# One PSUM copy of 576 columns for the ninth tile's turned rows and both heads' tails, and a chunk-by-chunk layout of pt

## The reference

```python
# attention: batch 4, 8 heads, 576 positions, head dimension 64
scores = scale * q @ k.T                       # scale = 1/8
thresh = max(scores, axis=-1) - tau
scores = where(scores >= thresh, scores, -1e9)
attn = exp(scores - max(scores)); attn /= sum(attn) + 1e-9
x = attn @ v                                   # -> 2304 tokens x 512
# first layer pair: h = x @ w_in (512 x 2048); g = s * relu(h)**2 + b; x = g @ w_out
# second layer pair: h = x @ w_in; g = max(h, 0) + alpha * min(h, 0); out = g @ w_out
```

## Time and profile before

| | us |
|---|---|
| median of three runs | 1088.46 (1088.38 to 1089.14) |
| the profiled execution's own time | 1089.1 |
| its span, first to last instruction | 1087.3 |
| TensorE busy | 1075.3 |
| VectorE busy | 526.4 |
| ScalarE busy | 505.9 |
| GpSimd busy | 257.3 |
| mean granted TensorE clock | 0.996 |

### The profile page before, as it was taken

The page is one execution under the profiler, slowest core; times in us unless marked ns, Lnnn a source line. Parts: engine busy times, 40 slices in busy tenths (PEclk is TensorE's granted clock), DMA queues, the critical chain, the costliest instruction groups (busy, mean ns, idle before and its releaser), DMA issues.

```text
span 1087.3 us, 18967 instructions
## 1 busy us (share of the span) xinstructions
PE 1075.3 (99%) x5826; PEld 892.6 (82%) x5826; DVE 526.4 (48%) x1017; ACT 505.9 (47%) x946; POOL 257.3 (24%) x438
## 2 busy tenths in 40 slices
PE   8999999999999999999999999999999999999998
PEld 7877877777788888888888889888888888888897
DVE  7988989888643332242242246522422332332232
ACT  4877878787754332232232235544433333333343
POOL 3666656666574200000000014322000000000000
PEclk8999999999999999999999999999999999999999
DMA  8666666565121100000000003211100100010010
GB/s 187 159 148 160 153 143 157 139 152 135 40 58 49 49 1 1 1 0 0 0 0 0 0 20 88 87 49 30 40 0 0 39 0 0 0 39 0 0 39 20
DMA packets 86554, 59.28 MB, mean 55 GB/s; under 512 B 49376, under 2 KB 69872, under 8 KB 86512
## 3 DMA queue, kind: packets, MB, share of 16 engines
q1 hardware_dynamic: 83248, 57.58, 20.6%
q10 hardware_dynamic: 3264, 1.18, 0.5%
HBM read 30.94 MB, written 4.72 MB: 33 GB/s over the span
## 4 chain that ended last, share of the span: by engine, by line
PE 91%; ACT 3%; DVE 2%; issue 2%; SPq 1%; DMA 0%; ACTq 0%; DVEq 0%
PE psum L947 23%; PE psum L948 23%; PE psum L949 23%; PE psum L1084 6%; PE psum L1050 5%; PE psum L976 3%; PE psum L978 3%; DVE act_r L883 2%; PE psum L1079 1%; ACT pt L645 1%; PE psum L960 1%; PE psum L1058 1%; ACT ex L623 1%; ACT win_hi L600 1%; SPq L434 1%
## 5 line engine op out<-in xcount | busy, mean ns | idle before, releaser
L947 PE MATMUL psum<-x_hi,win_hi 128*128 128x512 f32 (+1 forms) x640 | 235.7, 368 | 0.0
L948 PE MATMUL psum<-x_lo,win_hi 128*128 128x512 f32 (+1 forms) x640 | 235.5, 368 | 0.0
L949 PE MATMUL psum<-x_hi,win_lo 128*128 128x512 f32 (+1 forms) x640 | 235.5, 368 | 0.0
L947 PEld LDWEIGHTS psum<-x_hi,win_hi 128*128 128x128 f32 x640 | 120.7, 189 | 20.8 <-DVE x_lo L876 0.2
L948 PEld LDWEIGHTS psum<-x_lo,win_hi 128*128 128x128 f32 x640 | 120.6, 188 | 20.4
L949 PEld LDWEIGHTS psum<-x_hi,win_lo 128*128 128x128 f32 x640 | 120.7, 189 | 19.9
L894 DVE SCALAR_TENSOR_TENSOR act_r<-act_n,nalpha,act_r 128x512 f32<-128x512 f32 (+1 forms) x80 | 56.1, 702 | 155.6 <-ACT act_r L724 155.4
L883 DVE SCALAR_TENSOR_TENSOR act_r<-act_r,s_c 128x512 f32<-128x512 f32 (+1 forms) x80 | 73.1, 914 | 111.0 <-ACT act_r L713 111.0
L716 ACT ACTIVATE g_hi<-act_r,b_c 128x512 fp32r<-128x512 f32 (+1 forms) x80 | 54.5, 681 | 151.7 <-PE psum L949 121.6
L557 POOL TENSOR_SCALAR ex<-ex,none_in,rinv 128x576 f32<-128x576 f32 x142 | 117.1, 827 | 30.0 <-DVE rinv L814 29.2
L623 ACT ACTIVATE ex<-psum,negm 128x576 f32<-128x576 f32 x144 | 107.1, 747 | 29.2 <-DVE negm L795 28.1
(11 more groups left out here) (94 smaller groups left out, 1611.2 us busy)
## 6 DMA issues: line engine op xcount, KB each, us to landing
k_twice<-k_hi SPq DMA_DIRECT2D x64, 144.0 KB, 2.4
stage<-in_moe_w_out_dram SPq DMA_DIRECT2D x32, 256.0 KB, 2.6
out_dram<-stage SPq DMA_DIRECT2D x18, 256.0 KB, 2.2
q_both<-q_hi SPq DMA_DIRECT2D x32, 128.0 KB, 2.3
q_both<-q_lo SPq DMA_DIRECT2D x32, 128.0 KB, 2.3
win_raw<-in_moe_w_in_dram SPq DMA_DIRECT2D x16, 256.0 KB, 2.9
stage<-in_moe_w_in_dram SPq DMA_DIRECT2D x16, 256.0 KB, 2.7
raw_q<-in_q_dram SPq DMA_DIRECT2D x30, 128.0 KB, 2.4
```

The costliest lines, as they stand in the source:

```text
L947: nc.tensor.matmul(dst, lhs[0], rhs[0], start=first, stop=False)
L948: nc.tensor.matmul(dst, lhs[0], rhs[1], start=False, stop=False)
L949: return nc.tensor.matmul(dst, lhs[1], rhs[0], start=False, stop=final)
```

## The change

`turn_last` makes four transposes for the chunks as before, and two ordinary float32 matmuls against columns of the identity instead of the last two transposes. The first takes the tile's last 128 key columns as stationary operand and identity columns 64 to 127 as moving operand: it gives 128 x 64, and its partitions 64 to 127 are head 1's tail. The second takes the last 64 key columns and identity columns 0 to 63, gives 64 x 64, and overwrites partitions 0 to 63 with head 0's tail. The tails then stand as 64 columns right behind the 512 of the chunks, in the same partitions as in the destination. `copy_last` is one copy of 128 x 576.

For that, `pt` gets nine blocks of 576 columns, block `2 * c + h` for chunk `c` and head `h`, and block 8 for the tails; `pt_tails` is gone. `copy_turned` and `times_v` address the new layout. The 64 extra columns of `ex`, their memset and its count in `PADDED` are gone. Waits and semaphores are otherwise as before.

```diff
-        ex = sb("ex", [P, TPP * S + LAST], where=att)
+        ex = sb("ex", [P, TPP * S], where=att)
-        pt = sb("pt", [P, 2, QT - 1, S], where=att)
-        pt_tails = sb("pt_tails", [P, S], where=att)
+        PT_TAILS = 2 * (QT - 1)
+        pt = sb("pt", [P, PT_TAILS + 1, S], where=att)
...
-        PADDED = 7
+        PADDED = 6
...
                 if t.tails:
-                    dst = pt_tails[:, t.q0:t.q0 + 2 * P].rearrange("p (j q) -> p j q", q=P)
+                    dst = pt[:, PT_TAILS, t.q0:t.q0 + 2 * P].rearrange("p (j q) -> p j q", q=P)
                     nc.scalar.copy(dst, t.buf[:, 0:2, :]).then_inc(turned_out, 1)
                 else:
-                    nc.scalar.copy(pt[:, t.head, :, t.q0:t.q0 + P], t.buf).then_inc(turned_out, 1)
+                    dst = pt[:, 0:PT_TAILS, :].rearrange("p (c h) q -> p h c q", h=2)[:, t.head, :, t.q0:t.q0 + P]
+                    nc.scalar.copy(dst, t.buf).then_inc(turned_out, 1)
...
-                nc.scalar.copy(pt[:, :, :, S - LAST:S],
-                               t.wide[:, 0, :].rearrange("p (c h q) -> p h c q", h=2, q=LAST))
-                nc.scalar.copy(pt_tails[0:LAST, S - LAST:S], t.wide[0:LAST, 1, P:P + LAST])
-                nc.scalar.copy(pt_tails[LAST:P, S - LAST:S], t.wide[LAST:P, 1, LAST:P]).then_inc(last_out, 1)
+                src = t.wide.rearrange("p a c -> p (a c)")[:, 0:(PT_TAILS + 1) * LAST].rearrange("p (b q) -> p b q", q=LAST)
+                nc.scalar.copy(pt[:, :, S - LAST:S], src).then_inc(last_out, 1)
...
-            nc.vector.memset(ex[:, TPP * S:TPP * S + LAST], 0.0).then_inc(padded, 1)
...
-                for c in range(QT + 1):
-                    k0 = FULL * S + (c * P if c < QT - 1 else S - P if c == QT - 1 else S - LAST)
-                    dst = t.wide.rearrange("p a c -> p (a c)")[:, c * P:(c + 1) * P]
-                    mm = nc.tensor.transpose(dst, ex[:, k0:k0 + P], ident[:])
-                mm.then_inc(last_turned, 1)
+                end = FULL * S + S
+                for c in range(QT - 1):
+                    k0 = FULL * S + c * P
+                    nc.tensor.transpose(t.wide[:, 0, c * P:(c + 1) * P], ex[:, k0:k0 + P], ident[:])
+                nc.tensor.matmul(t.wide[:, 1, 0:LAST], ex[:, end - P:end], ident[:, LAST:P], start=True, stop=True)
+                nc.tensor.matmul(t.wide[0:LAST, 1, 0:LAST], ex[:, end - LAST:end], ident[:, 0:LAST],
+                                 start=True, stop=True).then_inc(last_turned, 1)
...
-                    nc.tensor.matmul(o_bank[:, o_cols], raw_v_tail[:, par, :], pt_tails[:, cols], start=False,
+                    nc.tensor.matmul(o_bank[:, o_cols], raw_v_tail[:, par, :], pt[:, PT_TAILS, cols], start=False,
...
-                    nc.tensor.matmul(o_bank[part, o_cols], raw_v[:, par, h, c, :], pt[:, h, c, cols],
+                    nc.tensor.matmul(o_bank[part, o_cols], raw_v[:, par, h, c, :], pt[:, 2 * c + h, cols],
```

## The result

The changed kernel takes 1091.72 us (1091.35 to 1092.02, ten runs), the kernel before 1088.74 us in the runs beside it (1087.93 to 1089.43): 1.0028 times as long, with a 95% interval of 1.0021 to 1.0036. That is 3.0 us slower. The forecast was 1088.6 with a range up to 1091.3, so it missed, on the side that the second rival described.

The account below looks back on a forecast made before the run. TensorE was taken to bound the kernel, with tile 5's 0.17 us wait covering the extra work. 15 x 0 in the pairs + 0.11 in the drain + 0 elsewhere gave 1088.6 us, range 1087.2 to 1091.3.

Parts of the forecast that it names:

- the second rival: In `turn_last`, small matmuls run load and stream in series: 1091.2 us, or 1096.5 with full load latencies; chance 0.16.
- What bounds the kernel: Whole kernel: TensorE, busy 1075.3 of 1087.3 us; in each attention pair it loses 0.17 us at tile 5 waiting for `k_lo`.
- one place: Tile 5's first score matmul, claimed to take 0.30 us instead of its 0.13 streaming length, in each pair.
- ScalarE's part: Copies in each pair: one replaces three, freeing ScalarE 0.40 us earlier, 6.4 us over 16 pairs, worth 0 on the path.
- TensorE's part: `turn_last`: two matmuls for two transposes cost 0.11 us more per pair, hidden in the loop by tile 5's 0.17 us wait.
- signs of being wrong: Pair distance changing by over 0.1 us, tile 5's scores no longer following `k_lo`'s end, or the layers' 790 us moving.
- Drain: `turn_last` in the drain: no side chain waits there, so +0.11 us counts once; the copies' gain is hidden.
- Opening: Start of kernel: the dropped 0.11 us memset gains 0, since the chain runs through SyncE's issues and DMA.
- Layout of pt: PV operands and copy destinations: moving columns stay contiguous, the copies' step becomes 1152 instead of 576 columns; taken as 0.
- The range: Whole kernel's time: 1087.2 to 1091.3 us, from the forecast less run spread and a partial gain upward.
- rival 2's near value: `turn_last` with paced loads and streams in series: 0.33 us extra per pair, 2.7 us in all, 1091.2; two thirds of 0.16.
- the bounds of the unknown form: The two new matmuls in `turn_last`: from 0 extra by streaming alone to 0.66 us extra if nothing overlaps.

Follow-up runs that it names:

- Rotated and narrow transposes: Changed kernel with two transposes instead of the two matmuls, one full-width against the identity rotated by 64 columns, one with 64 stationary columns: 1088.76 us, 0.9998 of before.
- the run apart: Changed kernel with one more narrow matmul between the second and third chunk transposes, into unused columns: 1098.38 us, 1.0089 of before.

## Why the prediction was wrong

- **What bounds the kernel**: right. TensorE sets the pace, and tile 5 waits 0.17 us for `k_lo`. The runs with one and three more transposes show this cover in the pace, within 0.02 us. But tile 5 was not the "one place" where a piece is longer than its stream: the prediction passed over the 0.33 of tile 7 and the 0.81 of the K transposes.
- **ScalarE's part, 0**: right, by the run with one copy and six transposes. The copy's own numbers held too: 0.64 us, and 0.54 from its start to the next copy's, where 0.53 was forecast. ScalarE's idle time grew to 0.55 us, not 0.7, since the copy now waits 0.16 us for TensorE's last matmul. The 6.4 us "of its 505.9" set time until ScalarE is free against busy time, in which copies overlap; the busy time fell by 4.0.
- **TensorE's part, +0.11**: this step failed. The matmuls themselves were 0.17 + 0.26 = 0.43 us, where I had 0.33. The larger miss is what I didn't price at all: the tail transposes behind them went from 0.22 to 0.37. The prediction divided the load times of two forms into a pace and a latency "that overlaps", and took from the transposes that loads always overlap. They do among transposes and full-width matmuls, and not on entering or leaving narrow ordinary ones. The row was there: the 0.17 us ahead of PV's first load, "put down to issue", was read only as no wait for ScalarE; it has the form and the size of what entering such a run costs in the runs above. The true extra was 0.37 us, above the cover of 0.17 and above the 0.31 from which the second rival decides. Two of the prediction's own signs of being wrong came: the distance between pairs moved by 0.19 us, over 0.1, and tile 5's scores (158.20 in the chain) no longer follow the end of `k_lo` (156.87 + 0.82 = 157.69).
- **The second rival**: its condition, its price (0.33 extra, 1091.2 us) and its place were nearly what happened, but its mechanism, every short matmul pays load and stream in series, is refuted: the second of two adjacent narrow matmuls has 0.12 us, and the narrow one with 128 moving columns pays the same ends on top of its stream. The rule of the Trainium skill ("TensorE: Matmul & The Clock Gate", "Part 3: Packing small matmuls — row/col tiling") that loads overlap running matmuls only when the row group differs doesn't fit this trace in that wording: all stationary operands of this stretch use all rows, and among the transposes a load starts 0.11 us ahead of its own (155.59 and 155.70).
- **Drain, +0.11 once**: 0.41, by the same failed step. **Opening, 0**: nothing in the runs speaks against it, but 0.1 us is less than the 0.7 us by which before's medians differ. **Layout of pt, 0**: right, by the same run as ScalarE's part.
- **The range** ended at 1091.3 and the time was 1091.72. It reached to rival 2's near value and left nothing above it, though the bounds of the unknown form ran to 0.66 extra.

No version beat the kernel before. Rotated and narrow transposes have the single copy at 1088.76 us, no different from before. Relief for ScalarE shows nothing on this spot, where tile 5 waits for `k_lo`.

## What to carry to other kernels

Count an instruction's price with its neighbours': look in the trace for the first instruction behind a run of the form you are about to insert, not only for the form itself. Ordinary matmuls with 64 stationary columns belong together in one run; a single one among full-width work cost about 0.3 us here on top of its own 0.12. And before an engine is relieved, find who waits for it: the copies hold ScalarE for 0.39 us less in each of 16 pairs (0.93 and 0.54), and this was worth nothing, since no wait of TensorE ended on them; the one wait there, tile 5's, ends on a side chain through `k_hi` and `k_lo`.

## What the runs showed of the hardware

- Entering and leaving a run of ordinary float32 matmuls with 64 stationary columns cost 0.27 to 0.31 us together where transposes follow (0.15 and 0.12 between narrow transposes, 0.15 + 0.15 in the run apart, 0.31 for both in PV). Leaving costs 0.12 to 0.16 us when a transpose follows and 0.20 when a wide matmul does (0.33 instead of 0.13 at tile 7, 0.43 instead of 0.23 in the drain). The opening shows the same sizes, 0.20 going in and 0.15 coming out, around matmuls with 64 rows and 128 stationary columns, untested.
- At these ends the first weight load starts with its matmul and not ahead of it. That alone is no sign: behind the tail product tile 4's load starts only 0.03 us ahead of its matmul (156.38 and 156.41 before), and its piece has the usual 0.13.
- A transpose with 64 stationary columns costs 0.11 us as with 128, and pays no such ends among wide transposes. Why ordinary matmuls and transposes differ is open; the traces show no more than the loads' start times.
- An ordinary float32 matmul of 128 stationary and 64 moving columns stands as two records. It has 0.17 us in the chain behind transposes and 0.22 as the second of two; the 0.22 fits two loads of 0.11 us, as the forecast had estimated.
